# Chain of decay products of the last batch cut in two: four chunks beside the third batch, two beside the last batch

## The chip, the cores and the metric

The kernel runs on one core of a Trainium2 chip. The metric is the device time of one execution in microseconds; a kernel's time is the median of several executions. One execution is recorded by the hardware profiler; its rows are what this text quotes.

## The reference, cut to what matters

Three layers one after the other: a linear attention with complex decay over 4 batches, 8 heads, 768 steps and 48 channels, a soft mixture of 8 experts, and a dense layer with a squared ReLU. The change is in the attention.

```python
mag = np.sqrt(a_re * a_re + a_im * a_im)
scale = np.minimum(mag, 0.999) / (mag + 1e-06)
a_re_n, a_im_n = (a_re * scale, a_im * scale)
for t in range(S):
    new_re = ar * S_re - ai * S_im        # ar, ai: the decay of step t, per channel
    new_im = ar * S_im + ai * S_re
    S_re, S_im = (new_re + kv, new_im)    # kv: outer product of k and v of step t
    y[:, :, t] = q[:, :, t] @ S_re
...
logits = x @ phi                          # mixture: softmax over tokens and over slots
h = np.maximum(slot_input[e] @ w1[e], 0.0); slot_out[e] = h @ w2[e]
...
h = np.maximum(x @ w_in, 0.0); return h * h @ w_out
```

## The kernel before, in words

**Tiling.** The 768 steps of a batch are 6 chunks of 128 steps; the chunks of all 4 batches are numbered n = 0 to 23 (batch n // 6). "The third batch" is n = 12 to 17, "the last batch" n = 18 to 23. Inside a chunk the steps are counted from its middle, 64 before and 64 after, so that two products of decays per chunk of up to 64 factors are wanted at every step. All chunks, both halves and all channels of a batch lie side by side in one tile (`big`), so one VectorE instruction does one step of the product for the whole batch.

**The chain of decay products of a batch b** (VectorE, named `big`, `tt`, `pexp`, `tu`, `gd` in rows), in this order:

1. `init_products` (L741 to L744).
2. 15 times `product_step` (L757, L759, L763: two products of 288 elements per partition, one sum), four blocks of 16 steps abreast.
3. 3 times `block_step` (L770 and L779 to L786: a copy, then six instructions of 576 elements), which multiplies a block by the end of the one before.
4. `square_sums` part 0 (L792, 1728 elements), `turn_factors` (L810 to L827, ten instructions of 15 or 30 elements that end in the tile `gd`), `square_sums` part 1 (L792, 576 elements).

ScalarE does the squares for step 4 (`product_squares`, L396), then a logarithm (`log_sums`, L402) and an exponential (`exponential`, L408), which give the inverse squared magnitudes. For the last batch the exponential of the first chunk (384 elements) comes first and that of the five others (1920 elements) after it. SyncE carries `gd` to `gst` with six DMAs (`stack_turns`, L275).

**One chunk n.** VectorE: `key_query(n, 0)` (L853, tile `xout`), `weigh(n)` (L835, multiplies by the exponential of ScalarE), `key_query(n, 1)` (L853), `build_turn(n)` (L865, needs `gst` of its batch). SyncE: `stack(n)`, six DMAs `stk<-xout` (L265). TensorE: `scores(n)` (L1093), `outputs(n-1)` (L1133, L1136), `next_state(n)` (L1111, L1114), `turn_x(n-1)` (L1162), `logits(n-1)` (L1150). Between them `keep_busy(k)` issues k matmuls whose result nobody reads (L1079, here 0.22 us each at the full clock). ScalarE: two copies of the scores' turned keys (`copy_kt`, L427), the copy of the outputs (`copy_y`, L439), of the state (`copy_state`, L433), and three more. VectorE masks the scores of chunk n-1 in two halves (`apply_mask`, L874) after `build_turn(n)`.

`scores(n)` waits for `stack(n)`, `build_turn(n)` and for both masks of chunk n-1, since it writes over the scores that they read:

```python
pe.wait_ge(stacked[n % NST], 96 * (n // NST + 1))
if turn:
    pe.wait_ge(rot_ready, turns(n) + 1)
for half in range(2):
    if n:
        pe.wait_ge(masked, 2 * (n - 1) + half + 1)
```

**What sets the order.** Each engine runs a program written out by hand; engines wait for each other only by semaphores. The loops run over a stage p and a chunk c of 6, with n = 6(p-1) + c: stage p works the chunks of batch p-1 and, on VectorE, the chain of batch p beside them. `parts` gives each piece of the chain a weight, and `go(p, x)` issues pieces until the share x of all weights is reached; `fill(p)` puts one small piece between two chunk instructions. So stage p = 3 (third batch) holds the whole chain of the last batch, and stage p = 4 (last batch) holds chunk work alone.

**After the attention.** The softmax sums, then `hidden(0)` to `hidden(3)` and `slot_outputs(0)` to `(3)` on TensorE (L1253, L1275), which read expert weights. Of those, 12 halves are loaded by ScalarE's queue (L351, `load_half`) during stages 3 and 4, and ten whole ones by SyncE's queue (L280, `load_w`), which comes after `stack(23)` in SyncE's program: five at once, three after the last outputs, two (k = 14 and 15, for `hidden(3)` and `slot_outputs(3)`) after `hidden(0)`. Behind them come `w_in` and `w_out`. Then the dense layer, 96 rounds of `gate` and `project`.

Of the kernel before, what the change touches and what calls it, by code (L numbers as in the profile page):

```python
# [10 lines left out]
ALU = mybir.AluOpType  # L11
# [31 lines left out]
def program(nc, a_all, xq_all, v_all, phi, w1, w2, w_in, w_out, out):  # L43
    with ExitStack() as ctx:
# [78 lines left out]
        EARLY = [W_AT.index(k) for k in range(6)]  # L123
        wt = [place(f"wt{k}", [P, KM * FE], offset=W_AT[k] * WT) for k in range(2 * NX)]
# [79 lines left out]
        C_SUM = C_BLOCK + 1  # L204
        C_TURN = C_SUM + 10
        C_ALL = C_TURN + 1


        BC = BL * NC
        PART = [(0, ([HP, TF], [1, (NB4 - 1) * BC])), ((NB4 - 1) * BC, ([HP, TF], [1, BC]))]  # L210

# [29 lines left out]
        def _(sp):  # L241
# [26 lines left out]
            def stack_turns(b):  # L268
                sp.wait_ge(chain, C_ALL * b + C_TURN)
                if b:  # L270
                    sp.wait_ge(rot_ready, (NC - 1) * b)
                for c in range(2):
                    for t in range(DT):
                        k = c * R1 + t
                        sp.dma_start(gst[k:k + DT * (DL - 1) + 1:DT],  # L275
                                     gd[:, c, t].rearrange("p c g -> p (c g)")).then_inc(g_stacked, 16)
# [67 lines left out]
        def _(act):  # L344
            act.wait_ge(consts, 2)

            def load_half(i):

                k, half = EARLY[i // 2], slice(i % 2 * KM * FE // 2, (i % 2 + 1) * KM * FE // 2)
# [38 lines left out]
            def product_squares(b, part, c):  # L388


                act.wait_ge(chain, C_ALL * b + (C_BLOCK if part else C_BLOCK - 7))
                if b >= 2 and part == 0:
                    act.wait_ge(weighed, NC * (b - 1))
                x, dims = PART[part]
                o = N_ if c else M_[b % 2]
                nc.scalar.activation(grid(o + x, *dims), grid(PL[b % 2] + c * PF + x, *dims), ACT.Square).then_inc(m_squares, 1)  # L396

            def log_sums(b, part):
                act.wait_ge(chain, C_ALL * b + (C_ALL if part else C_SUM))
                x, dims = PART[part]  # L400
                m = grid(M_[b % 2] + x, *dims)
                nc.scalar.activation(m, m, ACT.Ln).then_inc(m_log, 1)  # L402

            def exponential(b, c, count):

                act.wait_ge(m_log, 2 * (b + 1))
# [98 lines left out]
            for p in range(B + 1):  # L505
                for c in range(NC + 2 * (p == B)):
# [50 lines left out]
                    if c == NC - 1 and p < B:  # L557
                        exponential(p, 1, NC - 1)
# [9 lines left out]
                    if p < B - 1:  # L568
# [128 lines left out]
        def _(dve):  # L697
# [38 lines left out]
            def init_products(b):  # L736
                done, e = C_ALL * b, PL[b % 2]
                dve.wait_ge(signed, 3 * DT * (b + 1))
                dve.wait_ge(an_ready, DT * (b + 1))
                first = grid(e, [PT, 2 * DT], [2, NC])  # L740
                dve.tensor_copy(a0[:].rearrange("p c t x -> p (c t) x"), first).then_inc(chain, 1)  # L741
                dve.wait_ge(chain, done + 1)
                dve.memset(grid(e, [PT, DT], [2, NC]), 1.0).then_inc(chain, 1)
                dve.memset(grid(e + PF, [PT, DT], [2, NC]), 0.0).then_inc(chain, 1)  # L744
# [4 lines left out]
            def product_step(b, i, sums):  # L749

                done, e = C_ALL * b + C_INIT + 3 * (i - 1), PL[b % 2]
                dims = [[step_cols, tb], [2, NC]]
                t1 = bass.AP(tt, 0, [list(tt[:].ap[0]), [tb * NC, 2], [NC, tb], [1, NC]])
# [680 lines left out]
```

## Time and profile before

| | us |
|---|---|
| median of 3 executions | 627.73 |
| lowest and highest | 625.7, 629.93 |
| the profiled execution, device time | 626.63 |
| its span, first to last instruction | 624.9 |
| TensorE busy | 512.4 |
| VectorE busy | 401.3 |
| ScalarE busy | 351.6 |

The device time of the profiled execution is 1.73 us more than its span. A busy TensorE here includes the `keep_busy` matmuls. Times in rows are microseconds from the span's start. Busy time is a mean over stages with different limits, so that a stage has to be read by its own rows.

### The profile page before, as it was taken

What the parts mean: (1) busy time and instruction counts of PE and PEld (TensorE: products, weight loads), DVE (VectorE), ACT (ScalarE), POOL (GpSimd) and SP (SyncE); (2) the same over time, 40 slices, a digit from 0 to 9 for tenths busy, and PEclk for the clock granted to TensorE, in tenths of its full rate; (3) what the DMA queues carried; (4) which work ended last, traced back from release to release, by engine and by line L of the source; (5) the groups of instructions that cost most, each with busy time, mean ns of one, the idle gap of its engine ahead of it and who ended that gap; (6) DMA issues with size and microseconds to landing.
All of it is one profiled execution on the core that took longest, in us unless ns stands there. A gap on an engine that the chain in (4) does not pass through costs nothing.

```text
span 624.9 us, 11741 instructions
## 1 busy us (share of the span) xinstructions
PE 512.4 (82%) x4566; PEld 386.1 (62%) x4566; DVE 401.3 (64%) x660; ACT 351.6 (56%) x596; POOL 138.4 (22%) x120
## 2 busy tenths in 40 slices
PE   1000087995999959998999887999999999999997
PEld 1000045774676746776788633478888888888886
DVE  5699999899999999996552150399533333332322
ACT  5746732789577963357334311486555556565553
POOL 7000000000000000000000000066655555555553
PEclk9999987998999979999999998999999999999999
DMA  7400168473647456886877999200101001010101
GB/s 269 131 20 0 30 165 211 109 159 96 194 134 177 92 139 176 205 226 160 235 230 245 422 426 434 97 1 1 52 0 42 10 1 50 2 51 1 51 1 51
DMA packets 40455, 79.59 MB, mean 127 GB/s; under 512 B 7248, under 2 KB 28880, under 8 KB 38864
## 3 DMA queue, kind: packets, MB, share of 16 engines
q1 hardware_dynamic: 38672, 69.41, 37.3%
q10 hardware_dynamic: 1728, 9.44, 4.2%
q8 instruction: 36, 0.59, 0.4%
q14 instruction: 19, 0.16, 0.1%
HBM read 55.12 MB, written 4.72 MB: 96 GB/s over the span
## 4 chain that ended last, share of the span: by engine, by line
PE 63%; DVE 21%; ACT 6%; issue 5%; DMA 3%; SPq 1%; DVEq 0%; ACTq 0%
PE ps L1363 10%; PE ps L1359 10%; PE ps L1360 10%; PE ps L1093 7%; PE ps L1079 4%; PE ps L1333 3%; DVE tt L757 3%; DVE tt L759 3%; DVE big L763 3%; PE ps L1136 2%; PE ps L1133 2%; PE ps L1150 2%; PE ps L1253 2%; DVE big L731 2%; DMA stk<-xout 2%
## 5 line engine op out<-in xcount | busy, mean ns | idle before, releaser
L1058 DVE TENSOR_TENSOR qs<-rs 128x512 f32<-128x512 f32 x96 | 83.1, 865 | 118.4 <-ACT rs L630 118.4
L693 POOL TENSOR_TENSOR hlo<-qs,hhi 128x512 fp32r<-128x512 f32 x96 | 126.1, 1314 | 131.4 <-DVE qs L1058 127.2
L1079 PE MATMUL ps<-ident 128*32 128x512 bf16 x274 | 79.1, 398 | 61.2 <-DVE xout L853 61.2
L1359 PE MATMUL ps<-hhi,who 128*128 128x512 f32 x285 | 111.0, 389 | 0.0
L1360 PE MATMUL ps<-hhi,wlo 128*128 128x512 f32 x285 | 110.9, 389 | 0.0
L630 ACT ACTIVATE rs<-ps 128x512 f32<-128x512 f32 x96 | 57.4, 598 | 82.2 <-PE ps L1333 82.1
L1093 PE MATMUL ps<-stk 112*128 112x224 f32 (+1 forms) x384 | 78.8, 361 | 10.9 <-DMA stk<-xout 10.9
L1093 PEld LDWEIGHTS ps<-stk 112*128 112x128 f32 x384 | 69.9, 199 | 21.7 <-DMA stk<-xout 15.7
L1363 PE MATMUL ps<-hlo,who 128*128 128x512 f32 x285 | 80.5, 391 | 0.1
L685 POOL MEMSET sinz<- 128x768 f32 x1 | 0.7, 737 | 338.3 <-PE ps L1136 338.3
L1079 PEld LDWEIGHTS ps<-ident 128*32 128x32 bf16 x274 | 22.4, 98 | 85.4 <-DVE xout L853 61.5
L634 ACT ACTIVATE hhi<-rs 128x512 fp32r<-128x512 f32 x96 | 60.8, 633 | 3.1
L1363 PEld LDWEIGHTS ps<-hlo,who 128*128 128x128 f32 x285 | 53.2, 188 | 12.1 <-POOL hlo L693 1.3
L1359 PEld LDWEIGHTS ps<-hhi,who 128*128 128x128 f32 x285 | 53.5, 188 | 11.2
L1360 PEld LDWEIGHTS ps<-hhi,wlo 128*128 128x128 f32 x285 | 53.5, 188 | 11.1
L874 DVE TENSOR_TENSOR asb<-ps,mask 128x512 f32<-128x512 f32 x48 | 32.3, 684 | 22.3 <-ACT kts L427 13.8
L853 DVE TENSOR_TENSOR xout<-big,xq 128x768 f32<-128x768 f32 x48 | 45.7, 953 | 0.5
L427 ACT ACTIVATE kts<-ps 128x384 f32<-128x384 f32 x40 | 19.4, 485 | 46.0 <-PE ps L1093 46.0
L1333 PE MATMUL ps<-cst,ust 128*128 128x512 f32 x96 | 37.4, 392 | 0.2 <-DVE ust L1040 0.2
L1136 PE MATMUL ps<-asb,vr 128*48 128x128 f32 x384 | 35.5, 273 | 0.0
L1133 PE MATMUL ps<-stk,st 112*48 112x128 f32 x320 | 31.8, 276 | 0.0
L1150 PE MATMUL ps<-xts,phs 112*32 112x128 f32 x576 | 27.5, 288 | 2.0 <-issue 1.5
(160 smaller groups left out, 816.4 us busy)
## 6 DMA issues: line engine op xcount, KB each, us to landing
stk<-xout SPq DMA_DIRECT2D x144, 128.0 KB, 3.5
wt<-in_w SPq DMA_DIRECT2D x10, 1536.0 KB, 17.8
big<-in_a_all SPq DMA_DIRECT2D x12, 768.0 KB, 5.4
xq<-in_xq SPq DMA_DIRECT2D x24, 384.0 KB, 4.2
wt<-in_w ACTq DMA_DIRECT2D x12, 768.0 KB, 5.7
vr<-in_v_all SPq DMA_DIRECT2D x24, 192.0 KB, 4.3
out<-ost SPq DMA_DIRECT2D x5, 768.0 KB, 3.5
wins<-in_w_in SPq DMA_DIRECT2D x1, 3072.0 KB, 23.2
```

Source lines behind the costliest of these rows:

```text
L630: nc.scalar.activation(rs[:, i % NQS, :], ps[:, i % 2, :], ACT.Relu).then_inc(relu_ready, 1)
L634: nc.scalar.activation(hhi[:, i % NHS, :], rs[:, i % NQS, :], ACT.Square).then_inc(hi_ready, 1)
L693: pool.tensor_tensor(hlo[:, i % NHS, :], qs[:, i % NQS, :], hhi[:, i % NHS, :].bitcast(F32), ALU.subtract).then_inc(lo_ready, 1)
L853: dve.tensor_tensor(o, e, x, ALU.mult).then_inc(kq_ready, 1)
L1058: dve.tensor_tensor(qs[:, i % NQS, :], rs[:, i % NQS, :], rs[:, i % NQS, :], ALU.mult).then_inc(sq_ready, 1)
L1079: nc.tensor.matmul(ps[P - SL:P, bank, :], idb[:, 0:SL], idle, start=True, stop=True)
L1093: last = nc.tensor.matmul(ps[:, h // 2, h % 2 * SK:h % 2 * SK + cols], x[:, 0:CH], x[:, CH:CH + cols], start=True, stop=True)
L1136: last = nc.tensor.matmul(y, vr[:, n % NV, h * D:(h + 1) * D], asb[:, n % 2, h], start=(c == 0), stop=True)
L1333: nc.tensor.matmul(ps[:, i % 2, :], ust[:, f * P:(f + 1) * P], cst[:, t * TW:(t + 1) * TW], start=True, stop=True).then_inc(g_done, 1)
L1359: nc.tensor.matmul(accs[k], wh[k], hi, start=(f == 0), stop=False)
L1360: nc.tensor.matmul(accs[k], wl[k], hi, start=False, stop=False)
L1363: last = nc.tensor.matmul(accs[k], wh[k], lo, start=False, stop=(f == F2B - 1))
```

## The change

The chain of the last batch becomes two chains: chain 3 with chunks 0 to 3 of the batch (n = 18 to 21) in stage 3, and chain 4 with its chunks 4 and 5 (n = 22, 23) in stage 4, beside chunks 18, 19 and 20. Every function of the chain takes the chain's number g in place of the batch and works on `c1 - c0` chunks: a product of `product_step` has 192 elements in chain 3 and 96 in chain 4, one of `block_step` 384 and 192. SyncE issues `stack_turns` once more, for chain 4, behind `stack(20)`; `build_turn(21)` waits for it, since its factor reaches into chunk 22. In chain 4 the `turn_factors` come ahead of both `square_sums`. In stage 3 the `keep_busy(6)` ahead of the scores becomes `keep_busy(2)`. The order in which ScalarE loads the early weights changes.

```diff
+        LOAD_ORDER = EARLY[:3] + [EARLY[5], EARLY[3], EARLY[4]]
...
+        CHAINS = [(b, 0, NC) for b in range(B - 1)] + [(B - 1, 0, 4), (B - 1, 4, NC)]
+        NG = len(CHAINS)
+        SUMMED = [C_BLOCK + 1] * (NG - 1) + [C_BLOCK + 11]
+        TURNED = [C_BLOCK + 11] * (NG - 1) + [C_BLOCK + 10]
...
@@ SyncE
+                    if p == B and c == 2:
+                        stack_turns(B)
                     if c == NC - 1 and p < B:
                         stack_turns(p)
...
@@ ScalarE
+                    if p == B and c == 3:
+
+                        log_sums(B, 0)
+                        log_sums(B, 1)
+                        exponential(B, 4, 1)
+                        exponential(B, 5, 1)
                     if p == B and c < NC:
                         if c == 0:
-                            act.wait_ge(chain, C_ALL * B)
                             act.wait_ge(kq_ready, 2 * NC * (B - 1))
+                        elif c == 3:
+                            act.wait_ge(chain, C_ALL * NG)
                         load_half(NC + c)
...
-                        exponential(p, 1, NC - 1)
+                        exponential(p, 1, CHAINS[p][2] - 1)
...
+                    if p == B and c == 2:
+                        for part in range(2):
+                            product_squares(B, part, 0)
+                            product_squares(B, part, 1)
...
@@ VectorE
             def weigh(n):
                 b, c = divmod(n, NC)
-                dve.wait_ge(m_ready, 2 * b + 1 + (c > 0))
+                g = chain_of(n)
+                dve.wait_ge(m_ready, 2 * g + 1 + (c > CHAINS[g][1]))
...
                 if c == 0:
                     dve.wait_ge(g_stacked, 96 * (b + 1))
+                elif n == (B - 1) * NC + 3:
+                    dve.wait_ge(g_stacked, 96 * NG)
...
-                    between = p < B
+                    between = p < B or p == B and c < 3
+                    if p == B:
+
+                        mid, hi = [(1 + c + x) / 4 * LAST for x in (0.5, 1)]
...
+                        if n == NT - NC:
+
+                            go(p, 0.2)
                         weigh(n)
...
+                            if n == NT - NC:
+                                go(p, 0.35)
                             build_turn(n)
...
+                    if p == B and c == 3:
+                        go(p, 1)
...
@@ TensorE
-                        keep_busy(20 if n == NT - NC else 6 if full else 1)
+                        keep_busy(20 if n == NT - NC else 6 if n < NT - 2 * NC else 2 if full else 1)
```

**VectorE, first chunk of the last batch.** Before, between the two `key_query` of chunk 18 stands only `weigh` (`xq`), and behind them its turn, a maximum (`eb`) and the masks (`asb`) of chunk 17:

```order
L853 TENSOR_TENSOR xout<-big,xq 128x6x2x64
L835 TENSOR_TENSOR xq<-xq,big 128x384
L853 TENSOR_TENSOR xout<-big,xq 128x6x2x64
L865 TENSOR_TENSOR stk<-bm,gst 112x8x96
L880 TENSOR_REDUCE eb<-eb 96x1
```

Now (line numbers of the changed kernel) the fifth product step of chain 4, then `weigh(18)`, with the sixth around `key_query(18, 1)`:

```order
L792 TENSOR_TENSOR tt<-big 128x96
L794 TENSOR_TENSOR tt<-big 128x96
L798 TENSOR_TENSOR big<-tt 128x48x2
L875 TENSOR_TENSOR xq<-xq,big 128x384
L792 TENSOR_TENSOR tt<-big 128x96
L794 TENSOR_TENSOR tt<-big 128x96
L893 TENSOR_TENSOR xout<-big,xq 128x6x2x64
L798 TENSOR_TENSOR big<-tt 128x48x2
```

Nothing of the chunk's own work has changed; instructions of 96 elements stand between it.

**VectorE, chunks 21 and 22.** Before, behind the turn (`stk`) of chunk 21 come at once the masks of chunk 20, then chunk 22:

```order
L853 TENSOR_TENSOR xout<-big,xq 128x6x2x64
L865 TENSOR_TENSOR stk<-bm,gst 112x8x96
L874 TENSOR_TENSOR asb<-ps,mask 128x512 x2
L853 TENSOR_TENSOR xout<-big,xq 128x6x2x64
L835 TENSOR_TENSOR xq<-xq,big 128x384
L853 TENSOR_TENSOR xout<-big,xq 128x6x2x64
```

Now the two `square_sums` of chain 4 (`big<-big`) stand between the turn and the masks:

```order
L893 TENSOR_TENSOR xout<-big,xq 128x6x2x64
L907 TENSOR_TENSOR stk<-bm,gst 112x8x96
L828 TENSOR_TENSOR big<-big 128x6x24x4
L828 TENSOR_TENSOR big<-big 128x6x8x4
L916 TENSOR_TENSOR asb<-ps,mask 128x512 x2
L893 TENSOR_TENSOR xout<-big,xq 128x6x2x64
L875 TENSOR_TENSOR xq<-xq,big 128x384
L893 TENSOR_TENSOR xout<-big,xq 128x6x2x64
```

The sums wait for the squares of ScalarE, and the masks stand behind them.

**ScalarE, chunk 21.** Before, behind the two `copy_kt` of chunk 21 (`kts`) come a weight load, then the copy of the outputs and of the state:

```order
L427 ACTIVATE kts<-ps 128x384 x2
L351 DMA wt_77<-in_w 128x1536
L439 ACTIVATE xts<-ps 128x512
L433 ACTIVATE st<-ps 112x384
L454 ACTIVATE xsb<-ps 128x384
```

Now the squares of chain 4 stand behind the state copy of chunk 20, and the logarithms and exponentials, each kind with a table load, behind the `copy_kt` of chunk 21:

```order
L454 ACTIVATE st<-ps 112x384
L415 ACTIVATE big<-big 128x6x24x4 x2
L415 ACTIVATE big<-big 128x6x8x4 x2
L501 ACTIVATE sums<-ps 96x385
L475 ACTIVATE xsb<-ps 128x384
L467 ACTIVATE eb<-ps 96x128
L448 ACTIVATE kts<-ps 128x384 x2
L422 ACT_TABLE_LOAD
L422 ACTIVATE big<-big 128x6x24x4
L422 ACTIVATE big<-big 128x6x8x4
L429 ACT_TABLE_LOAD
L429 ACTIVATE big<-big 128x192x2 x2
```

Eight instructions of chain 4 and two table loads have come into ScalarE's program of the last batch: the four squares ahead of `copy_kt(21)`, the rest behind it.

## Rows read from the trace of the kernel before

**Rows 1.** Stretches: us, busy PE, PEld, DVE, ACT, POOL, clock, DMA share, GB/s.
```profile
232.00:242.00 10.00, 10.00 (x127) 7.60 (x128) 9.90 (x21) 3.55 (x9) 0.00 (x0) 1.00 0.70 185
...
325.00:334.00 9.00, 9.00 (x145) 7.87 (x145) 4.09 (x6) 3.10 (x8) 0.00 (x0) 1.00 0.59 167
```

**Rows 2.** Timeline of TensorE: start, duration, line, tiles, count, [idle before, releaser].
```profile
253.34 3.29 PE L1093 MATMUL ps<-stk 112*128 112x224 f32 x16 [0.86 <-DMA stk<-xout]
...
285.93 0.75 PE L1150 MATMUL ps<-xts,phs 112*32 112x128 f32 x15 [1.50 <-issue]
...
298.20 3.29 PE L1093 MATMUL ps<-stk 112*128 112x224 f32 x16
...
307.22 3.29 PE L1093 MATMUL ps<-stk 112*128 112x224 f32 x16
...
315.07 3.29 PE L1093 MATMUL ps<-stk 112*128 112x224 f32 x16
...
324.81 3.29 PE L1093 MATMUL ps<-stk 112*128 112x224 f32 x16
...
333.55 3.29 PE L1093 MATMUL ps<-stk 112*128 112x224 f32 x16
```

**Rows 3.** Chain that ended last, 190 to 350: start, us, what.
```profile
274.18 0.87 PE ps L1079 x4
```

**Rows 4.** Timeline of VectorE, third and last batch.
```profile
225.73 0.46 DVE L757 TENSOR_TENSOR tt<-big 128x288 f32<-128x288 f32 x1
226.10 0.45 DVE L759 TENSOR_TENSOR tt<-big 128x288 f32<-128x288 f32 x1
226.59 0.46 DVE L763 TENSOR_TENSOR big<-tt 128x288 f32<-128x288 f32 x1
...
245.10 0.95 DVE L853 TENSOR_TENSOR xout<-big,xq 128x768 f32<-128x768 f32 x1
...
258.81 0.75 DVE L779 TENSOR_TENSOR tt<-big,pexp 128x576 f32<-128x576 f32 x1
...
288.10 0.56 DVE L835 TENSOR_TENSOR xq<-xq,big 128x384 f32<-128x384 f32 x1 [2.50 <-ACT big L408]
...
321.36 0.96 DVE L853 TENSOR_TENSOR xout<-big,xq 128x768 f32<-128x768 f32 x1
```

**Rows 5.** Timeline of ScalarE, end of the third batch and last batch.
```profile
281.61 1.28 ACT L402 ACT_TABLE_LOAD   x1
282.90 1.64 ACT L402 ACTIVATE big<-big 128x1728 f32<-128x1728 f32 x1
284.76 0.68 ACT L402 ACTIVATE big<-big 128x576 f32<-128x576 f32 x1 [0.22 <-DVE big L792]
...
287.51 0.55 ACT L408 ACTIVATE big<-big 128x384 f32<-128x384 f32 x1
...
322.61 0.49 ACT L433 ACTIVATE st<-ps 112x384 f32<-112x384 f32 x1 [1.07 <-PE ps L1114]
...
328.14 0.49 ACT L427 ACTIVATE kts<-ps 128x384 f32<-128x384 f32 x1 [1.02 <-PE ps L1093]
```

**Rows 6.** SyncE's queue: one `stack`, the last two, the weight loads.
```profile
246.08 3.78 SPq L265 DMA_DIRECT2D stk<-xout  x6
...
322.35 14.36 SPq L265 DMA_DIRECT2D stk<-xout  x12
336.75 27.51 SPq L280 DMA_DIRECT2D wt<-in_w  x10
```

**Rows 7.** Timeline of TensorE, `hidden(2)` and `hidden(3)`.
```profile
366.52 2.78 PE L1253 MATMUL ps<-wt,sinz 128*32 128x512 f32 x24
...
378.32 4.18 PE L1253 MATMUL ps<-wt,sinz 128*32 128x512 f32 x24 [5.86 <-issue]
```

**Rows 8.** Stretches of TensorE alone: us, PE busy, granted clock, DMA share, GB/s.
```profile
225.00:226.00 1.00, 0.00 (x0) 0.50 0.25 55
...
378.00:380.00 2.00, 1.68 (x8) 0.50 1.03 436
```

More of the change, by code:

```diff
@@ L203, in program, with chain_of, some @@
         C_BLOCK = C_SCAN + 7 * (NB4 - 1)
-        C_SUM = C_BLOCK + 1
-        C_TURN = C_SUM + 10
-        C_ALL = C_TURN + 1
+        C_ALL = C_BLOCK + 12
         BC = BL * NC
-        PART = [(0, ([HP, TF], [1, (NB4 - 1) * BC])), ((NB4 - 1) * BC, ([HP, TF], [1, BC]))]
+        CHAINS = [(b, 0, NC) for b in range(B - 1)] + [(B - 1, 0, 4), (B - 1, 4, NC)]
+        NG = len(CHAINS)
+        SUMMED = [C_BLOCK + 1] * (NG - 1) + [C_BLOCK + 11]
+        TURNED = [C_BLOCK + 11] * (NG - 1) + [C_BLOCK + 10]
+        def chain_of(n):
+            return n // NC + (n // NC == B - 1 and n % NC >= 4)
+        def some(off, c0, c1, part):
+            blocks = 1 if part else NB4 - 1
+            return grid(off + part * (NB4 - 1) * BC + 2 * c0, [HP, TF], [2 * NC, blocks * BL // 2], [1, 2 * (c1 - c0)])
         def turns(n):
@@ L266, in stack, with stack_turns @@
                           .then_inc(stacked[n % NST], 16)
-            def stack_turns(b):
-                sp.wait_ge(chain, C_ALL * b + C_TURN)
+            def stack_turns(g):
+                b, c0, c1 = CHAINS[g]
+                sp.wait_ge(chain, C_ALL * g + TURNED[g])
                 if b:
                     sp.wait_ge(rot_ready, (NC - 1) * b)
+                c0 = max(c0 - 1, 0)
                 for c in range(2):
@@ L347, in load_half @@
             def load_half(i):
-                k, half = EARLY[i // 2], slice(i % 2 * KM * FE // 2, (i % 2 + 1) * KM * FE // 2)
+                k, half = LOAD_ORDER[i // 2], slice(i % 2 * KM * FE // 2, (i % 2 + 1) * KM * FE // 2)
                 src = (w2 if k % 2 else w1)[k // 2].rearrange("p a b -> p (a b)")
@@ L386, in root, with product_squares, log_sums, exponential @@
                 overshoot(b, t)
-            def product_squares(b, part, c):
-                act.wait_ge(chain, C_ALL * b + (C_BLOCK if part else C_BLOCK - 7))
+            def product_squares(g, part, c):
+                b, c0, c1 = CHAINS[g]
+                act.wait_ge(chain, C_ALL * g + (C_BLOCK if part else C_BLOCK - 7))
                 if b >= 2 and part == 0:
                     act.wait_ge(weighed, NC * (b - 1))
-                x, dims = PART[part]
                 o = N_ if c else M_[b % 2]
[L396 to L401, printed above, removed]
+                nc.scalar.activation(some(o, c0, c1, part), some(PL[b % 2] + c * PF, c0, c1, part),
+                                     ACT.Square).then_inc(m_squares, 1)
+            def log_sums(g, part):
+                b, c0, c1 = CHAINS[g]
+                act.wait_ge(chain, C_ALL * g + (C_ALL if part else SUMMED[g]))
+                m = some(M_[b % 2], c0, c1, part)
                 nc.scalar.activation(m, m, ACT.Ln).then_inc(m_log, 1)
-            def exponential(b, c, count):
-                act.wait_ge(m_log, 2 * (b + 1))
+            def exponential(g, c, count):
+                b = CHAINS[g][0]
+                act.wait_ge(m_log, 2 * (g + 1))
                 x = grid(M_[b % 2] + 2 * c, [HP, TF], [2 * NC, HC // 2], [1, 2 * count])
@@ L842, in key_query @@
                 else:
-                    dve.wait_ge(chain, C_ALL * b + C_BLOCK)
+                    dve.wait_ge(chain, C_ALL * chain_of(n) + C_BLOCK)
                     dve.wait_ge(ld_xq[n % NXQ], 16 * (n // NXQ + 1))
@@ L914, in go @@
                     one(b)
+            LAST = (ends[TURNS + 3] + 0.5) / ends[-1]
             def shift(p, x):
@@ L953, in _ @@
                         norm2(p + 1, c - 1)
-                    if p < B:
+                    if between:
                         go(p, mid)
+                    if p == B and c == 3:
+                        go(p, 1)
                     if 0 < p < B and c == NC - 1:
@@ L979, in _ @@
                             one(p)
-                    if p < B:
+                    if between:
                         go(p, hi)
```

102 lines of the change are left out of this document (55 added, 47 removed).

## The prediction

> **What bounds the kernel now.** I read the stretches first. Inside the third batch's stage both engines are full: VectorE 9.90 of 10 us, TensorE 10.00 of 10. Inside the last batch's stage TensorE is full (9.00 of 9) and VectorE has 4.09 of 9 [rows 1]. So VectorE work that leaves the third batch helps only as far as TensorE can follow, and work that comes to the last batch finds about 5 us a chunk free.
>
> Then the timeline of TensorE [rows 2]. `scores(14)` starts at 253.34 after a wait of 0.86 us for the stack's DMA, the longest and last of three (the others stand ahead of 12 and 13), so VectorE and the DMAs behind it set the pace up to there. Later no such wait is left: TensorE itself sets the pace, and part of its work is `keep_busy`. Four such matmuls take 0.87 us [rows 3]. In the last batch the scores start at 298.20, 307.22, 315.07, 324.81 and 333.55 [rows 2].
>
> Last, SyncE: the weight loads start at 336.75, directly behind the last stack [rows 6], and `hidden(3)` on TensorE sits idle 5.86 us until 378.32 [rows 7]. It reads the last but one of these loads, and the DMA engines are saturated there (share 1.03, 436 GB/s) [rows 8]. So between the attention and the dense layer not TensorE's own time decides, but when that stream of weights began. A TensorE that comes up to 5.86 us later loses nothing there.
>
> **Part 1: what the third batch gains.** VectorE: an instruction of 288 elements takes 0.46 us, one of 576 takes 0.75 [rows 4], which is 0.29 us for 288 elements or 0.10 for 96. In chain 3, 45 product instructions lose 96 elements (4.5 us), 18 block instructions lose 192 (3.6), the sums lose 576 and 192 (0.8): about 9 us less VectorE in six chunks, 1.2 to 1.5 a chunk. The bound from below: were an instruction's time fixed and not by its elements, the gain would be 0.
>
> TensorE: four `keep_busy` fewer ahead of each of `scores(13)` to `(17)`, 5 x 0.87 = 4.3 us; those ahead of `scores(12)` stood before a DMA wait and bring nothing. To that come the DMA waits ahead of `scores(13)` and `(14)`, which VectorE now makes shorter (1.2 us in all), and the stall of 1.50 us at 285.93 [rows 2], in which `logits` waited for the state copy behind ScalarE's squares and logarithms; these have two thirds of their elements now, and I leave 0.6 of it. Sum: 4.3 + 1.2 + 0.9 = 6.4 us, all on the path. `scores(18)` then starts near 291.9 instead of 298.20 (-6.3). Its data are no later: chain 3 ends 7 us earlier on VectorE, the 2.50 us wait of `weigh(18)` for ScalarE [rows 4] is filled by five product steps of chain 4, and `xout(18)` is written at about 284.3. From the end of the second `xout` to the scores it takes 253.34 - 246.05 = 7.3 us [rows 2, 4], so 291.6. Bounds of this part: 0 (nothing shrinks and the clock drops, below) and -6.4.
>
> **Part 2: what chain 4 adds to chunks 18 to 20.** 45 instructions of 96 elements. By the same slope one lasts 0.26 us, and starts 0.17 us after an independent one. Dependent ones of 288 stand 0.49 apart [rows 4], so 0.29 here: 0.75 us a step, 11.2 us in all. 18 of 192 elements at 0.27 apart make 4.9, copies, turn and sums 3. Some 19 us against about 5 us free in each chunk and the lead that VectorE has won. I followed VectorE instruction by instruction: `xout(19)` complete at 295.0, plus 7.2 gives `scores(19)` at 302.2, where TensorE alone would come at 301.0 (-5.0 against before). `xout(20)` is complete at 302.5, masks of 19 at 306.8, so `scores(20)` starts at 302.2 + 7.85 = 310.05 (-5.0). So far chain 4 costs 1.3 us.
>
> **Part 3: the squares stand ahead of the masks.** Chain 4's squares wait on ScalarE behind the state copy of chunk 20, and its sums stand on VectorE ahead of the masks of chunk 20, for which `scores(21)` waits. Before, the state copy of 20 starts 322.61 - 315.07 = 7.5 us after `scores(20)` [rows 2, 5]. Behind it now: the copy 0.5, four squares 1.6 (576 elements took 0.68, [rows 5]), the last sum 0.3, both masks ready from there: first mask end 0.65, gaps 0.2. Together 10.8 instead of 9.74 us. `scores(21)` starts at 320.9, against 324.81. The second door is as late: SyncE issues the six DMAs of `stack_turns` (3.8 us, as the six of a stack [rows 6]) from 309.8 and so the stack of 21 only from 313.6, which gives 320.9 too. I take 321.0 (-3.8).
>
> **Part 4: the exponentials of chain 4 come late.** This is the term that decides. `weigh(22)` needs the first exponential of chain 4. Its logarithm stands on ScalarE behind `copy_kt(21)`, which needs `scores(21)`. Counted from the start S of `scores(21)`: the second `copy_kt` starts 328.14 - 324.81 = 3.3 later and ends at 3.8 [rows 2, 5]. Then table load 1.28, logarithms 0.6 and 0.3, table load 1.28, exponential of 384 elements 0.55 [rows 5], gaps 0.1: S + 7.9. `weigh` 0.5, `xout` 0.95: S + 9.4. Stack 7.1: S + 16.5. So `scores(22)` starts at 337.5, where before it started at 333.55: before, `xout(22)` was complete at 322.3, ahead even of `scores(21)` [rows 4]. Here the gain of 3.8 us turns into a loss of 4.0. Queued behind the waiting `weigh(22)` on VectorE are the turn of 22, the masks of 21 and the whole of chunk 23; behind the logarithms on ScalarE the output copy of 20, for which `turn_x(20)` waits some 1.5 us.
>
> In these columns a table load occupies ScalarE for 1.28 us and the logarithm starts 1.29 us after it [rows 5]. The Trainium skill, "ScalarE: Activation LUTs", *What ACT_TABLE_LOAD costs*, adds a drain of about 1380 ns to every switch, 2.66 us in total; by that, two switches would put `scores(22)` another 2.8 us later, at 340.3. The trace shows no such gap at this load, so the sum goes by 1.28.
>
> **Part 5: the clock.** TensorE now idles about 6 us ahead of `scores(22)`. With the engine idle from 221 on, the granted clock was 0.50, that is 1.2 GHz, at 225 [rows 8], and ahead of `hidden(3)` an idle of 5.86 us left it at 0.50: 24 matmuls took 4.18 us instead of 2.78 [rows 7, 8], a loss of 1.4. I put 1.5 behind `scores(22)`. `scores(23)` and all of TensorE's path to `hidden(3)` are then 4.0 + 1.5 = 5.5 later.
>
> **Part 6: what of it arrives at the end.** `xout(22)` at S + 9.4, its turn, a maximum and the masks of 21 to S + 11.9, chunk 23 to S + 14.3, its stack issued by S + 18.7: the weights start at 339.7 instead of 336.75, 3.0 later. TensorE reaches `hidden(3)` at 372.46 + 5.5 = 378.0, the weights come at 378.32 + 3.0 = 381.3: still the later of the two. The idle there shrinks from 5.86 to 3.3 us, and with it part of the loss of 1.4 to the low clock; I take half, -0.8. Net +2.2 us. Behind that nothing is changed.
>
> The profiled execution is 626.63 us, its span 624.9 plus 1.73 around it. The sum gives 626.63 + 2.2 = 628.8. It lies 1.1 below the median of 627.73, from which the forecast is counted: 629.9, rounded to 630.
>
> **The rivals.**
>
> *The weights hide it all* (626 to 628.5). If the stack of 23 is issued faster than in 5 us and the clock stays up at `hidden(3)`, the shift is +1.6 - 1.4, near 0. For it: the last twelve stack issues needed 14.36 us where twice 3.78 would be 7.6, so they waited [rows 6]. Against: they waited for chunk 23, which is late now. Time 627.7.
>
> *Slower: the lead never reaches chunk 21* (634 to 637). The mechanism is the start of the third batch's stage. TensorE was idle there and at 0.50 until 231 [rows 8]; four of the `keep_busy` that bring it back ahead of `scores(12)` are gone. The Trainium skill, "TensorE: Matmul & The Clock Gate", *What's actually happening*, has it that the default is the low clock and activity releases it, which speaks against this cut. If `scores(12)` runs at 1.2 GHz it takes up to 3.3 us more; masks and scores behind it follow. From there on every us that S stands later goes through parts 4 to 6 undiminished. With S at 324.8, no lead, the weights start at 343.5, +6.8 us, less 0.8: about 633.8; with 2 us more of low clock 636. It decides once the lead at `scores(21)` is under 0.5 us. Against: part 1 rests on instructions that are simply gone.
>
> *Faster: the lead carries to the end* (621 to 625). Were the exponentials of chain 4 ready for `weigh(22)`, `scores(22)` would stand at S + 8.7 + 1.6 = 331.3, 2.2 ahead of before, and the weights start 2 to 4 us earlier: 624.5; with the whole lead of 6.3 us, 621.4. Against it is the order of the instructions: logarithms behind `copy_kt(21)` on ScalarE, for which `scores(21)` is a condition.
>
> **How the numbers follow.** Forecast 0.5 (its own range 627 to 634), hidden 0.2, slower rival 0.2, faster rival 0.1. A measurement of this kernel tells about 1% from no change, 6.3 us: 621.4 and 634.0. Over 634.0 lie two thirds of the slower rival and a tenth of the forecast: 0.17. Under 621.4 a third of the faster one, with something for the unforeseen: 0.05. The range from 624.5 to 636 takes in S from 318.5 to 324.8 and leaves out less than two in ten.
>
> **What would show it.** Right: `scores(18)` near 292, `scores(21)` near 321, a wait of `weigh(22)` for ScalarE's exponential of 5 us or more, `scores(22)` 16 to 17 us behind `scores(21)`, a granted clock of 0.5 at `scores(22)`, weights from about 339.7, an idle of TensorE ahead of `hidden(3)` of 2 to 4 us. Wrong: a `weigh(22)` that does not wait; a `scores(12)` at the low clock; or a `hidden(3)` that starts without a wait, for then the whole 5.5 us count. Instructions of 96 elements that last more than 0.3 us would sink part 2.

## The result and the profile after

The changed kernel takes 645.09 us, median of 6 executions (642.79 to 647.78), against 627.59 (625.70 to 629.93) for the kernel before on the same chip: a ratio of 1.0281, 95% interval 1.0251 to 1.0310. That is 17.5 us slower, and 9 us beyond the upper end of the range. The profiled execution takes 642.79 us with a span of 641.0, which is 16.1 more than 624.9 before; the difference is explained on these two (the profiled execution is the fastest of the six).

TensorE's timeline, all six `scores` of the last batch, the first and third of the third batch and `hidden(2)`, `hidden(3)` (they answer to [rows 2, 7]):

```profile
231.36 5.51 PE L1148 MATMUL ps<-stk 112*128 112x224 f32 x16 [1.51 <-DMA stk<-xout]
...
253.13 3.10 PE L1148 MATMUL ps<-stk 112*128 112x224 f32 x15 [1.17 <-DMA stk<-xout]
...
294.83 3.29 PE L1148 MATMUL ps<-stk 112*128 112x224 f32 x16
...
308.34 6.26 PE L1148 MATMUL ps<-stk 112*128 112x224 f32 x16 [4.42 <-DMA stk<-xout]
...
319.16 3.29 PE L1148 MATMUL ps<-stk 112*128 112x224 f32 x16
...
333.31 5.73 PE L1148 MATMUL ps<-stk 112*128 112x224 f32 x16 [4.33 <-DMA stk<-xout]
...
352.54 6.34 PE L1148 MATMUL ps<-stk 112*128 112x224 f32 x16 [6.29 <-DMA stk<-xout]
...
365.32 2.05 PE L1148 MATMUL ps<-stk 112*128 112x128 f32 x16
...
388.56 2.78 PE L1308 MATMUL ps<-wt,sinz 128*32 128x512 f32 x24
...
395.85 2.78 PE L1308 MATMUL ps<-wt,sinz 128*32 128x512 f32 x24 [1.34 <-issue]
```

Read the bracket and the duration together. In the last batch the same 16 matmuls take 3.29 us where they follow other work at once, and 5.7 to 6.3 behind a wait. `scores(19)`, `(21)` and `(22)` each wait more than 4 us for a stack's DMA; before, there was no such wait in this batch. The granted clock says the rest. The first and the last stretch lie inside slow scores; the middle one answers to the second of [rows 1] (columns as there):

```profile
309.00:311.00 2.00, 2.00 (x7) 1.82 (x6) 0.00 (x0) 0.00 (x0) 0.00 (x0) 0.50 1.13 162
325.00:334.00 9.00, 4.67 (x104) 3.53 (x104) 3.09 (x5) 3.69 (x10) 0.00 (x0) 0.86 0.79 183
...
353.00:355.00 2.00, 2.00 (x7) 1.78 (x7) 0.00 (x0) 0.00 (x0) 0.00 (x0) 0.50 1.18 163
```

In the middle stretch TensorE was busy 9.00 of 9 us before; now 4.67. A clock of 0.50 is 1.2 GHz.

SyncE's issues, which answer to [rows 6] (start, time from the first to the last of the group):

```profile
297.56 3.84 SPq L280 DMA_DIRECT2D stk<-xout  x6
304.55 3.80 SPq L280 DMA_DIRECT2D stk<-xout  x6
318.84 3.77 SPq L292 DMA_DIRECT2D gst<-gd  x6
322.72 3.85 SPq L280 DMA_DIRECT2D stk<-xout  x6
345.28 8.50 SPq L280 DMA_DIRECT2D stk<-xout  x12
...
353.82 32.48 SPq L297 DMA_DIRECT2D wt<-in_w  x10
```

Issuing costs what it did before, 3.8 us for six. What has changed is the time from issue to landing, which each row gives as the shortest, the median and the longest of a stack's six DMAs. The stacks of chunks 19, 20 and 21, before:

```profile
DMA to landing us min/median/max: 2.9/3.5/4.8
DMA to landing us min/median/max: 3.3/3.7/5.1
DMA to landing us min/median/max: 3.2/3.5/5.4
```

And now:

```profile
DMA to landing us min/median/max: 2.8/6.0/7.5
DMA to landing us min/median/max: 5.4/5.8/7.3
DMA to landing us min/median/max: 6.0/6.1/7.3
```

ScalarE's queue names what runs beside them. In the changed kernel two weight halves go out inside the issue of a stack (298.46 in that of 19, 322.79 in that of 21); before, the half of chunk 18 went out at 301.88, when all six DMAs of stack 19 (296.93 to 300.7) had been issued:

```profile
298.46 0.34 ACTq L370 DMA_DIRECT2D wt<-in_w  x1
...
322.79 0.34 ACTq L370 DMA_DIRECT2D wt<-in_w  x1
```

Inside the stack of 19 the landing changes where the half comes. Its first DMA, issued at 297.56, ahead of the half, and its second, whose issue runs from 298.2 to 298.8, across that of the half:

```profile
DMA to landing us min/median/max: 2.8/2.8/2.8
DMA to landing us min/median/max: 5.6/5.6/5.6
```

The four behind them took 5.9, 6.1, 6.6 and 7.5 us. The stack of 20 holds no half in its issue; it was issued 6.1 us behind one and was slow all the same.

VectorE and ScalarE around `weigh(22)`, the wait that was forecast:

```profile
323.81 0.96 DVE L907 TENSOR_TENSOR stk<-bm,gst 112x768 f32<-112x768 f32 x1 [2.67 <-DMA gst<-gd]
...
343.70 0.56 DVE L875 TENSOR_TENSOR xq<-xq,big 128x384 f32<-128x384 f32 x1 [12.24 <-ACT big L429]
```

```profile
339.08 0.49 ACT L448 ACTIVATE kts<-ps 128x384 f32<-128x384 f32 x1 [1.89 <-PE ps L1148]
339.59 1.28 ACT L422 ACT_TABLE_LOAD   x1
340.88 0.94 ACT L422 ACTIVATE big<-big 128x576 f32<-128x576 f32 x2
341.83 1.28 ACT L429 ACT_TABLE_LOAD   x1
...
343.13 0.98 ACT L429 ACTIVATE big<-big 128x384 f32<-128x384 f32 x2
```

The order of these rows is the one forecast, and so is its engine: `copy_kt(21)`, load, logarithms, load, exponentials, `xq`. The wait of 12.24 us is long because `scores(21)` itself is 12.3 us behind its forecast, and because `copy_kt(21)` follows it at the low clock.

### The profile page after: what moved, and what is told of

Same layout as the page of the kernel before. It is cut to its first block, busy times and chain, and to the rows that moved or that the text cites. A ratio compares the mean times of both kernels' runs of the same rounds, so it can differ in the third digit from the quotient of the medians.

```text
span 641.0 us, 11795 instructions
## 1 busy us (share of the span) xinstructions
PE 513.5 (80%) x4542; PEld 390.7 (61%) x4542; DVE 409.4 (64%) x741; ACT 354.8 (55%) x606; POOL 139.0 (22%) x120
## 4 chain that ended last, share of the span: by engine, by line
PE 55%; DVE 21%; ACT 8%; DMA 7%; issue 5%; SPq 4%; ACTq 0%; DVEq 0%
PE ps L1418 10%; PE ps L1414 10%; PE ps L1415 10%; PE ps L1148 7%; DMA stk<-xout 6%; SPq L280 3%; PE ps L1388 3%; DVE tt L792 3%; DVE big L798 3%; DVE tt L794 3%; PE ps L1134 2%; DVE xout L893 2%; DVE big L763 2%; PE ps L1308 2%; PE ps L1330 2%
## 5 line engine op out<-in xcount | busy, mean ns | idle before, releaser
L1134 PE MATMUL ps<-ident 128*32 128x512 bf16 x250 | 73.5, 398 | 61.2 <-DVE xout L893 61.2
L1148 PE MATMUL ps<-stk 112*128 112x224 f32 (+1 forms) x384 | 86.7, 386 | 29.6 <-DMA stk<-xout 29.6
L1148 PEld LDWEIGHTS ps<-stk 112*128 112x128 f32 x384 | 76.3, 216 | 40.6 <-DMA stk<-xout 34.8
L1134 PEld LDWEIGHTS ps<-ident 128*32 128x32 bf16 x250 | 20.0, 98 | 82.9 <-DVE xout L893 61.5
L1414 PEld LDWEIGHTS ps<-hhi,who 128*128 128x128 f32 x285 | 53.5, 188 | 11.2
L798 DVE TENSOR_TENSOR big<-tt 128x288 f32<-128x288 f32 (+2 forms) x75 | 29.7, 396 | 1.6
## 6 DMA issues: line engine op xcount, KB each, us to landing
wt<-in_w SPq DMA_DIRECT2D x10, 1536.0 KB, 14.1
wins<-in_w_in SPq DMA_DIRECT2D x1, 3072.0 KB, 18.7
```

The source lines that it names most:

```text
L798: dve.tensor_tensor(grid(spot(e, i), [PF, 2], *dims), t1, t2, ALU.add).then_inc(chain, 1)
L1134: nc.tensor.matmul(ps[P - SL:P, bank, :], idb[:, 0:SL], idle, start=True, stop=True)
L1148: last = nc.tensor.matmul(ps[:, h // 2, h % 2 * SK:h % 2 * SK + cols], x[:, 0:CH], x[:, CH:CH + cols], start=True, stop=True)
L1414: nc.tensor.matmul(accs[k], wh[k], hi, start=(f == 0), stop=False)
```

## The experiments

Medians; "before" is the kernel before on the same chip, 626.66 us for the first five, 626.82 for e5 to e8, 627.11 for e9 to e12, 626.81 for the last three. All edits are to the changed kernel, except in e2 and e7. The changed kernel itself was timed on its own, 17.5 us over the kernel before; so the runs are compared by how far each stands over the kernel before of its own group.

**Is it the cut of `keep_busy`?** e1 puts the 6 back, e2 makes the cut alone, in the kernel before.

```diff
-keep_busy(20 if n == NT - NC else 6 if n < NT - 2 * NC else 2 if full else 1)
+keep_busy(20 if n == NT - NC else 6 if full else 1)
```

> The changed kernel with the six keep-busy matmuls ahead of the scores of the third batch restored (its own cut to two undone). In the changed kernel scores(12) ran 5.51 us at 1.2 GHz instead of 3.29, and TensorE stood at 294.83 at scores(18) where 291.9 was predicted. Theory A (the late exponentials, the slow landing of two stacks and the low clock that follows each wait make the loss; the cut is a side matter): scores(12) takes 3.3 us again, 2.2 us won there, up to 0.87 us lost ahead of each of scores(15) to (17); the time stays within 2 us of 645. Theory B (the cut lets the clock fall and that is what costs): the time falls by 8 us or more, and no scores of the last batch runs at 1.2 GHz.

> The kernel before with one part of the change alone: two keep-busy matmuls instead of six ahead of the scores of the third batch, the chain whole. Theory A: scores(12) at 1.2 GHz, +2.2 us, about 0.87 us less ahead of each scores where TensorE sets the pace; VectorE is full in this stage, so little of that is kept: within 2 us of 627.6. Theory B: 633 or more.

e1: 645.20, ratio 1.0303 [1.0254, 1.0353]. e2: 625.67, ratio 0.9990 [0.9968, 1.0012]. With the 6 back `scores(12)` runs at the full clock:

```profile
232.28 3.29 PE L1148 MATMUL ps<-stk 112*128 112x224 f32 x16
```

yet nothing is won, and in e2 `scores(12)` takes 5.77 us and nothing is lost. In these two kernels the cut is neutral: the low clock at `scores(12)` is real, but `scores(14)` then waits for its stack anyway (1.17 us in the change, 2.66 in e2). It need not stay neutral once the other losses are mended: see e11 and e15 below.

**Is it the place of the exponentials?** e3 moves logarithms and exponentials of chain 4 ahead of both `copy_kt(21)`.

```diff
+if p == B and c == 3:
+    log_sums(B, 0); log_sums(B, 1); exponential(B, 4, 1); exponential(B, 5, 1)
 if 0 <= n < NT and has_turn(n):
     copy_kt(n, 0)
```

> The changed kernel with chain 4's two logarithms and two exponentials ahead of the two score copies of chunk 21 on ScalarE instead of behind them; nothing else. Theory A: the 12.24 us wait of weigh(22) falls to 2 to 4 us (sums at 329.3, then 4.2 us of ScalarE), scores(22) no longer waits for its stack (PE-paced, near 344.5 instead of 352.5) and runs at 2.4 GHz: scores(23) 8 to 11 us earlier; at hidden(3) the weights become the limit again, so 6 to 10 us at the end: 635 to 639. Rival (SyncE and the DMA engines are what makes scores(22) late, not ScalarE's order): scores(22) still waits 4 us or more for its stack, the time falls by less than 4 us.

637.85, ratio 1.0192 [1.0151, 1.0234]: 11.2 us over the kernel before instead of 17.5, so 6.3 are won. TensorE and `weigh(22)` of e3:

```profile
307.89 5.94 PE L1148 MATMUL ps<-stk 112*128 112x224 f32 x16 [5.66 <-DMA stk<-xout]
...
332.88 5.40 PE L1148 MATMUL ps<-stk 112*128 112x224 f32 x16 [4.68 <-DMA stk<-xout]
...
345.22 3.29 PE L1148 MATMUL ps<-stk 112*128 112x224 f32 x16 [1.43 <-DMA stk<-xout]
```

```profile
333.12 0.56 DVE L875 TENSOR_TENSOR xq<-xq,big 128x384 f32<-128x384 f32 x1 [2.43 <-ACT big L429]
```

The wait of `weigh(22)` falls from 12.24 to 2.43 us and `scores(22)` is fast again. `scores(19)` and `(21)` are as they were, each with its wait and its low clock.

**Are the landings late because of the weight halves?** e4 holds the six halves of the last batch back to chunks 22 and 23.

```diff
-load_half(NC + c)
+if c >= 4:
+    for i in range(3):
+        load_half(NC + 3 * (c - 4) + i)
```

> The changed kernel with the six weight halves that ScalarE's queue issues during the last batch held back: none beside chunks 18 to 21, three each at chunks 22 and 23. In the changed kernel the last stack DMA of chunks 19 and 21 took 7.5 and 7.3 us to land, with a weight half (786 KB) issued in the same microseconds, against 3.5 us in the median before. Theory A (the half and the stack share the DMA engines): stacks 19, 20 and 21 land in under 4.5 us, scores(19) waits under 1.5 us and runs at 2.4 GHz (6 to 7 us won there), scores(21) too is earlier by 3 us or more on top; weigh(22) still waits about 8 to 12 us. The time falls by 4 to 11 us, less what three halves more in the last stream cost (about 1.8 us each where the weights bound hidden(3)). Rival (the landing is slow for another reason, such as xq and v loads or the number of descriptors): landings stay over 5.5 us, the time does not fall.

640.79, ratio 1.0225 [1.0183, 1.0268], 14.1 us over the kernel before. The stacks of 19, 20 and 21 land as before:

```profile
DMA to landing us min/median/max: 2.8/3.6/4.8
DMA to landing us min/median/max: 2.9/3.5/4.2
DMA to landing us min/median/max: 2.9/3.4/4.4
```

```profile
306.94 3.29 PE L1150 MATMUL ps<-stk 112*128 112x224 f32 x16 [1.59 <-DMA stk<-xout]
314.79 3.29 PE L1150 MATMUL ps<-stk 112*128 112x224 f32 x16
...
326.01 3.29 PE L1150 MATMUL ps<-stk 112*128 112x224 f32 x16 [1.41 <-DMA stk<-xout]
...
342.94 6.14 PE L1150 MATMUL ps<-stk 112*128 112x224 f32 x16 [6.43 <-DMA stk<-xout]
...
388.63 4.98 PE L1332 MATMUL ps<-wt,hts 128*32 128x384 f32 x32 [5.33 <-DMA wt<-in_w]
```

`scores(21)` starts 7.3 us earlier than in the change, and two of three slow scores are gone. `scores(22)` stands 16.93 us behind `scores(21)`, where the prediction said 16.5. Of these gains little reaches the end: the halves are now missing behind the attention, the last row above. So this run shows the cause by its landings, not by its time. The loads `xq<-in_xq` and `vr<-in_v_all`, which SyncE issues behind a stack, are still there, so they alone do not make the landings late.

**What do late halves cost by themselves?** e7 makes the edit of e4 in the kernel before; e6 is e3 and e4 together; e11 is e6 with `keep_busy(6)`.

> The kernel before with the six weight halves of the last batch held back in the same way (three each at chunks 22 and 23), the chain whole: what the edit costs by itself. The attention is paced by TensorE, so it gains nothing there; the last stream carries 2.4 to 3.1 MB more, at 430 GB/s 5 to 7 us, and hidden(3) waited 5.86 us for it already: 631 to 635. If it stays at 627, the halves were free and the second edit's cost in the changed kernel has another cause.

> The changed kernel with both edits at once: chain 4's logarithms and exponentials ahead of the score copies of chunk 21, and the six weight halves of the last batch held back to chunks 22 and 23. Alone the first gave 637.9 and the second 640.8. If they act at separate places (one at scores(22), the other at the stacks of 19 and 21), scores(23) stands 13 to 17 us earlier than in the changed kernel, near 349 to 352, but the halves make hidden(1) and slot_outputs wait, so the end gains little more: 632 to 637. Rival (they are two views of one wait): scores(23) not earlier than 354.

> The changed kernel with early logarithms and exponentials, late weight halves (both edits gave 638.7 together) and six keep-busy matmuls again in the third batch. In the run of the two edits scores(12) and scores(14) ran at 1.2 GHz; the six put 2 to 5 us of that back and cost up to 2.6. 635 to 639. If it falls under 633, the cut of the keep-busy matmuls has a part in the loss that its own undoing did not show.

e7: 634.06, ratio 1.0121 [1.0099, 1.0144], 7.2 us for the delay alone, with an attention as long as before (`scores(12)` to `(23)` 111.6 us, 111.4 before). Taken off e4's 14.1, that would leave 6.9 us for the split with its stacks alone, an estimate that holds only if the two costs add. Behind it TensorE waits twice for weights instead of once:

```profile
377.92 4.24 PE L1277 MATMUL ps<-wt,hts 128*32 128x384 f32 x32 [5.83 <-issue]
386.23 2.78 PE L1255 MATMUL ps<-wt,sinz 128*32 128x512 f32 x24 [3.48 <-issue]
```

e6: 638.65, ratio 1.0174 [1.0145, 1.0203], over the range I had given (632 to 637), with `scores(23)` at 354.71 instead of 349 to 352; in its third batch `scores(14)` too waits (3.23 us) and runs slow (5.87 us). e11: 635.09, ratio 1.0127 [1.0101, 1.0152], 8.0 us over the kernel before, where e7 is 7.2 over it. With exponentials early, stacks without weight halves beside them and `keep_busy` as before, the split chain costs next to nothing at the end, and gains nothing either. In the attention it still costs: from `scores(12)` to `scores(23)` are 115.5 us in e11, 134.0 in the change, 111.4 before.

**What does the low clock cost?** e5 puts `keep_busy` matmuls into three waits; e12 into the first two, e13 into the last.

```diff
+keep_busy({19: 20, 21: 20, 22: 28}.get(n, ...))   # e12: {19: 20, 21: 20}; e13: {22: 28}
```

> The changed kernel with more keep-busy matmuls where TensorE waited idle: 20 ahead of scores(19) and scores(21), 28 ahead of scores(22), instead of 1. Theory A (each wait costs once as idle time and a second time as scores at 1.2 GHz): scores(19), (21) and (22) take 3.3 us each instead of 6.26, 5.73 and 6.34, the score copies of chunk 21 come 2 us earlier and with them weigh(22); scores(23) is 6 to 9 us earlier, and the end 4 to 8 us (637 to 641). Rival (the clock is a symptom only, the waits would stretch to the same ends): less than 2 us.

> The changed kernel with 20 keep-busy matmuls ahead of scores(19) and scores(21) alone, none added ahead of scores(22). With all three places the profiled execution took 639.3 and three others 645, so this asks again in more rounds. Theory A (low clock costs twice 2.7 us at these two places and a third time through what waits for them): 638 to 642. Rival (the clock costs nothing in most executions, since the stack of the next chunk, not TensorE, sets the pace): 644 to 646.

> The changed kernel with 28 keep-busy matmuls ahead of scores(22) alone. 20 ahead of (19) and (21) gave 638.9, all three places 644.8 in the median and 639.3 in the profiled execution. Theory A (the clock at scores(22) is a loss like the others): 3 us at scores(22), and up to that at the end: 641 to 644. Rival (the 28 delay TensorE there or keep it from the work of chunk 20 and 21, and that took back the gain of the other two): 645 or more.

e12: 638.88, ratio 1.0190 [1.0165, 1.0216], 11.8 us over the kernel before, so 5.7 are won. e13: 645.22, ratio 1.0298 [1.0262, 1.0335], nothing, though in its profile `scores(22)` runs at the full clock:

```profile
354.22 3.29 PE L1148 MATMUL ps<-stk 112*128 112x224 f32 x16 [1.08 <-DMA stk<-xout]
```

The low clock at `scores(19)` and `(21)` is on the path, since masks, squares and exponentials follow from them. That at `scores(22)` is not: the weight stream behind `stack(23)` is by then the later one (in e13 TensorE idles 2.75 us ahead of `hidden(3)`, in the change 1.34). e5 should have been as good as e12 and was not: 644.79, ratio 1.0268 [1.0224, 1.0312]. Its profiled execution took 639.29 us and shows three fast scores; its other three took 644.6 to 645.5. What these did differently no profile shows; it stays open, and with it how much a warm clock is worth there.

**Do the gains add?** e8 joins early exponentials, warm matmuls at 19 and 21 and weight halves ahead of the copies; e14 is e3 with e12; e15 adds `keep_busy(6)` to e14.

> The changed kernel with the logarithms and exponentials ahead of the score copies of chunk 21, the weight half of each chunk of the last batch ahead of its score copies instead of behind them (so that it is issued before the stack of the next chunk, not with it), and 20 keep-busy matmuls ahead of scores(19) and (21). If late exponentials, slow landings and the low clock make up the loss, scores(23) stands near 345 to 350 and the end at 628 to 634. If the squares and the six DMAs of the turn ahead of chunk 21's stack hold it up, scores(21) still stands 11 us or more behind scores(20), and nothing below 627 comes out. A time clearly under 626.7 would say that the split pays once these are gone.

> The changed kernel with the logarithms and exponentials of chain 4 ahead of the score copies of chunk 21 (637.9 alone) and 20 keep-busy matmuls ahead of scores(19) and (21) (638.9 alone), the weight halves as in the change. If the two losses are separate, 630 to 634, and scores(23) 12 to 16 us earlier than in the changed kernel. If the stacks that land beside weight halves hold it, 635 or more.

> The same with six keep-busy matmuls again in the third batch, which keep scores(12) at 2.4 GHz. Third batch as long as before less 2 us, last batch as in the kernel with early exponentials and a warm clock: within 2 us of that kernel. Under 626 would say that the split of the chain pays once the waits are mended; I expect 630 to 635.

e8: 636.17, ratio 1.0124 [1.0075, 1.0174], over the 628 to 634 that I had given. Its profiled execution took 629.64 us and has no slow score in the last batch (`scores(23)` at 348.98); its other three took 636.1 to 636.4, and as in e5 no profile shows why. e14: 637.71, ratio 1.0172 [1.0116, 1.0228], a miss: no better than e3. e15: 634.29, ratio 1.0120 [1.0097, 1.0143]. e3 and e12 win 6.3 and 5.7 us each and 6.6 together. The profile of e14 shows two places where the next door was as late, the turn's DMAs and again a stack:

```profile
330.31 0.96 DVE L907 TENSOR_TENSOR stk<-bm,gst 112x768 f32<-112x768 f32 x1 [10.05 <-DMA gst<-gd]
```

```profile
346.48 6.19 PE L1148 MATMUL ps<-stk 112*128 112x224 f32 x16 [4.75 <-DMA stk<-xout]
```

There the stacks of 22 and 23 landed in 5.8 to 7.6 us; a weight half (336.26) had gone out just ahead of the first DMA (336.38).

Twice the six `keep_busy` matmuls went back into a kernel with other losses mended. e11 stands 8.0 us over the kernel before where e6 stands 11.8 over it, e15 7.5 where e14 stands 10.9. The intervals of each pair overlap, so a gain is not shown, but a cost of the cut in such a kernel is not ruled out either.

**Is it where the chain is cut?** e9 cuts at five chunks and one; e10 adds early exponentials and `keep_busy(6)`.

```diff
-[(B - 1, 0, 4), (B - 1, 4, NC)]
+[(B - 1, 0, 5), (B - 1, 5, NC)]
```

> One size changed: the last batch's chain cut at five chunks and one instead of four and two. Chain 4 holds chunk 23 alone (48 elements a product), its turn, squares, sums, logarithm and exponential all come one chunk later (beside chunk 21, logarithm behind the score copies of chunk 22), and two weight halves move behind it. Theory A (what costs is a fixed latency: ScalarE's logarithms behind the score copies of the chunk before, the stack behind them, the landing beside a weight half, each followed by the low clock): the long wait moves from weigh(22) to weigh(23), stays 8 to 12 us, and the loss is nearly the same, 640 to 648. Rival (the amount of work in chain 4 is what the last batch cannot hold): half the elements gain 3 us or more of the loss a chunk, the time falls to 632 to 638.

> Cut at five chunks and one, the logarithm and exponential ahead of the score copies of chunk 22, six keep-busy matmuls again in the third batch. The last chunk's stack then waits for sums, logarithm and exponential only. Theory A: weigh(23) waits under 4 us, some 6 to 9 us won against the cut at five alone; 632 to 639, still over 626.8 as long as the stacks of 19 to 21 land beside weight halves.

e9: 636.51, ratio 1.0150 [1.0121, 1.0179], against my own expectation of 640 to 648 and in the rival's range; the long wait did move to `weigh(23)`, but to 6.64 us. e10: 635.59, ratio 1.0134 [1.0098, 1.0170]; there `weigh(23)` waits only 2.86 us, yet `scores(23)` still waits 6.52 for its stack. In e9 the waits at 19 and 21 are 1.11 us and none; one long one is left:

```profile
353.26 3.78 PE L1149 MATMUL ps<-stk 112*128 112x128 f32 x16 [7.44 <-DMA stk<-xout]
```

In e9 most of stack 19 goes out ahead of the half: it is issued at 297.87, the half at 300.82, since `scores(18)` starts at 297.19 and ScalarE follows it (297.56, 298.46 and 294.83 in the change). It lands in a median of 3.5 us. By its median no version of the split came below the kernel before. The changed order of the early weights was in every one of them and is not tested by itself; in the change's profile TensorE waits for a weight only at `hidden(3)`, whose load is not one of these.

## Why the prediction was wrong

The forecast of the profiled execution was 628.8; it is 642.79. The step that failed is the time from a stack to its scores, taken as a constant 7.2 us (part 2) and 7.3 us (part 3): it was 10.8 and 10.6, and each of these two waits brought a low clock that the sum did not have. The end follows the weight stream in both kernels: `hidden(3)` starts 41.6 us after the first SyncE weight load before, 42.0 now. That load starts at 353.82 where 339.7 was forecast, 14.1 us late; the rest (the idle and the clock at `hidden(3)`) is within 0.3 us. So all is in those 14.1.

**Part 1 (third batch, -6.3): right sign, half the size.** `scores(18)` is at 294.83, -3.4, so 2.9 us are missing, nearly all of them up to `scores(14)`, which stands at 253.13 against 253.34 before. I took out all DMA waits ahead of `scores(14)`; one of 1.17 stands there. Its stack was issued at 243.52, 0.26 us behind a weight half, and landed in 5.5 us. The rival's mechanism, `scores(12)` at the low clock, came true (5.51 us), and e1 and e2 show that it decided nothing in these two kernels. (The terms of this part add to 6.4, and I went on with 6.3.)

**Part 2 (chain 4 beside 18 to 20, +1.3): the failed step.** VectorE was followed rightly: `xout(19)` ends at 297.5, which is the forecast 295.0 plus most of the 2.9 above. Behind it I added "7.2" from a row of the third batch [rows 2, 4], as a constant. It was 10.8: from the last issue at 300.77 the DMA took 7.53 us. TensorE's lead was part of the trouble. ScalarE issues the half of chunk 18 with the second `copy_kt(18)`, so it came forward with `scores(18)`, by 3.4 us (301.88 to 298.46), while stack 19 went back by 0.6 (296.93 to 297.56); now both went out in the same microseconds. The stack of 21 goes out 3.6 us after the start of `scores(20)`, behind the turn's DMAs; before, it went out 0.9 us ahead of it, and so ahead of the half that follows that score. e4 moves only the halves and shows what they cost: the 10.8 us are 8.1 there (`xout(19)` ends at 298.85), and from `scores(18)` to `(21)` it takes 29.8 us, where 29.1 was forecast and the change took 38.5. The busy share of the DMA engines does not show the trouble. In the change, while this stack landed, and before, while the last of its stack 19 landed in 4.8 us:

```profile
305.00:307.00 2.00, 0.00 (x0) 0.00 (x0) 2.00 (x7) 0.00 (x0) 0.00 (x0) 1.00 1.08 152
```

```profile
301.00:303.00 2.00, 2.00 (x25) 1.43 (x25) 0.86 (x2) 0.60 (x2) 0.00 (x0) 1.00 1.16 163
```

Both are full, and both move far less than the 436 GB/s at 1.03 of [rows 8]. What differs is when the half comes: before, behind all six DMAs of stack 19, now behind the first. Why those behind it take so much longer no row shows, nor why stack 20 is slow 6.1 us behind a half, when before it went out 3.6 us behind one and landed in a median of 3.7 us. The Trainium skill, "DMA: Bandwidth & Descriptors", *Issuing engines are not separate DMA queues*, says that transfers from different issuing engines run on the same 16 DMA engines and interleave. The trace agrees: two queues, and a median landing of 6.0 us instead of 3.5.

**Part 3 (`scores(21)` at 321.0): both doors as named, one heavier.** Turn DMAs are issued at 318.84 and the stack of 21 only behind them, as said. It then took 10.6 us to the scores instead of 7.3, for the same cause (7.7 in e4): 333.31.

**Part 4 (`scores(22)` at S + 16.5): right mechanism.** It is S + 19.2, of which 2.4 us are `copy_kt(21)` behind slow scores (5.8 us after S instead of 3.3). Where these were fast, in e4, it is S + 16.9. The table load took 1.28 us with the logarithm 1.29 us behind it, so the sum by the row stands and the one with a drain falls.

**Part 5 (the clock, +1.5 once): undersized.** I priced one wait. There were three, of 4.3 to 6.3 us, and each made the 16 matmuls 2.4 to 3.1 us longer; by e12 the first two cost 5.7 us at the end. In e4 the waits at 19 and 21 are 1.59 and 1.41 us and neither score is slow, so this loss too follows from the landings. The third, the one I priced, costs nothing there (e13).

**The sum.** From forecast to fact, at `scores(21)`: third batch 2.9, landing of stack 19 3.2 more than forecast (interval 18 to 19 of 13.51 against 10.3), clock at 19 3.0 (10.82 against 7.85), landing of stack 21 3.2 (14.15 against 10.95). Together 12.3. From there to the weight loads 20.5 us instead of 18.7, mostly the clock at 21: 1.8. That makes the 14.1.

**Part 6 (the weights hide some): its rule held, its size did not matter.** The idle ahead of `hidden(3)` shrank to 1.34 us, not 3.3, and 1.4 us of low clock were saved, not 0.8. But a cover for TensorE is none for a delay of the weights themselves, and the delay went into `stack(23)`, which they stand behind.

**The rivals.** The slower one named a lead that does not reach chunk 21. It did not, but by DMA contention and not by the start of the third batch; I held `scores(21)` at 324.8 as the worst and it was 333.3. I bounded every new instruction from both sides and left out that the changed time of an issue changes what it meets. (By its own terms, the chance over 634.0 adds to 0.18, not 0.17.)

## What to carry to other kernels

A landing time read from an unloaded row is a price for that alignment only: when a change moves an engine that feeds one DMA queue against an engine that feeds another, forward or back, look up which loads of the other queue will now go out in the same microseconds, and give the landing the range from alone to shared. Where TensorE has no slack, count every wait of some 4 us twice, once for itself and once for the fp32 matmuls behind it at 1.2 GHz; shorter waits are not safe either (in e11 one of 1.87 us was followed by 16 matmuls of 4.93, in e4 one of 2.65 by 16 of 3.29). And when several late steps overlap, test the repairs together, since the gains of single ones do not add.

## What was not expected of the hardware

Six small DMAs of a stack (median 3.5 us to land when alone) took a median of 4.8 to 6.3 us when a weight half of 768 KB went out within 0.3 us of the first of them (chunks 14, 16, 17 and 21 of the changed kernel: 5.5, 6.3, 4.8 and 6.1; stacks at 243.52, 263.46, 273.43 and 322.72, halves at 243.26, 263.54, 273.17 and 322.79). Before, a half that went out 1.8 us ahead (263.75, stack at 265.53) left the median at 3.6, as did one 1.5 us ahead in e1 (241.97, stack at 243.48). In these rows a shift of some 2 us decides.

`keep_busy` matmuls put into a wait paid at `scores(19)` and `(21)` (20 each in e12: 3.3 us instead of 5.7 to 6.3, 5.7 us at the end) and paid nothing at `scores(22)` (28 in e13), each counted against the kernel before on its own chip.
